# The first half expert's weights beside the last early products, and a new order of token blocks

## The reference, cut to what matters

```python
x = attention(q, k, v, beta)            # reshaped to 3072 tokens x 384
logits = x @ w_gate; P = exp(logits - logits.max())
for _ in range(8):                      # "Sinkhorn rounds"
    P /= P.sum(1, keepdims=True) + 1e-09
    P /= P.sum(0, keepdims=True) + 1e-09
    P *= N / E
for e in range(8):                      # w1[e]: 384 x 1024, w2[e]: 1024 x 384
    out += P[:, e:e+1] * (np.maximum(x @ w1[e], 0) @ w2[e])
h = out @ w_in                          # second layer, 384 x 2048
out = (h * sigmoid(1.702 * h)) @ w_out
```

## Time and profile before

| what | us |
|---|---|
| median of 3 runs (lowest to highest) | 2574.24 (2572.38 to 2574.74) |
| the profiled execution, whole time | 2572.69 |
| its span (first to last instruction) | 2570.9 |
| TensorE busy | 2466.6 (96%) |
| VectorE, ScalarE, GpSimd busy | 1013.1, 663.9, 841.4 |
| share of the last chain on TensorE | 73% |

### The profile page before, as it was taken

One profiled execution on the slowest core, in us unless ns is written; L12 is line 12 of the kernel. 1 busy time (PEld: TensorE's weight loads), 2 busy tenths in 40 slices (PEclk: granted clock), 3 DMA queues, 4 the chain that ended last, 5 costly groups with the idle time before them and its releaser, 6 DMA issues.

```text
span 2570.9 us, 42139 instructions
## 1 busy us (share of the span) xinstructions
PE 2466.6 (96%) x17923; PEld 2362.1 (92%) x17923; DVE 1013.1 (39%) x2181; ACT 663.9 (26%) x1454; POOL 841.4 (33%) x753
## 2 busy tenths in 40 slices
PE   5889999999849999999999999999999999999999
PEld 4778888888749999999999999999999999999999
DVE  5776666663513333333333333333333333333332
ACT  3344444443311111111111111111111122222222
POOL 5545555552060232033113302321331131443432
PEclk9999999999979999999999999999999999999999
DMA  2113323332220111011001101110110010000001
GB/s 78 45 63 102 107 95 108 102 105 75 68 98 2 49 50 32 18 49 50 25 25 50 50 16 35 50 42 8 50 50 25 25 50 1 25 13 13 13 19 56
DMA packets 96378, 124.58 MB, mean 48 GB/s; under 512 B 5184, under 2 KB 82240, under 8 KB 96192
## 3 DMA queue, kind: packets, MB, share of 16 engines
q1 hardware_dynamic: 96192, 121.90, 14.3%
HBM read 91.99 MB, written 29.88 MB: 47 GB/s over the span
## 4 chain that ended last, share of the span: by engine, by line
PE 73%; issue 1%; DMA 1%; POOL 0%; DVE 0%; ACT 0%; SPq 0%; ACTq 0%; DVEq 0%; POOLq 0%
PE bank L1218 39%; PE bank L1189 32%; PE bank L181 1%; PE bank L1121 1%; DMA w_raw<-in_moe_w 0%; PE bank L1167 0%; POOL w_hl L1043 0%; POOL w_hl L1037 0%; DMA h_early<-h_out 0%; DVE h_raw L1327 0%; DVE x_rest L1333 0%; ACT x_rest L1247 0%; PE bank L1107 0%; PE bank L1225 0%; ACT h_out L191 0%
## 5 line engine op out<-in xcount | busy, mean ns | idle before, releaser
L1218 PE MATMUL bank<-w_hl,h_hl 128*128 128x384 f32 x5760 | 1021.5, 334 | 34.1 <-issue 34.1
L1218 PEld LDWEIGHTS bank<-w_hl,h_hl 128*128 128x128 f32 x5760 | 1001.9, 188 | 34.4 <-issue 34.4
L1189 PE MATMUL bank<-x_rest,w_hl 128*128 128x384 f32 x4320 | 783.3, 338 | 0.0
L1189 PEld LDWEIGHTS bank<-x_rest,w_hl 128*128 128x128 f32 x4320 | 763.9, 187 | 0.0
L1371 DVE SCALAR_TENSOR_TENSOR x_tok<-bank,route,x_tok 128x384 f32<-128x384 f32 x384 | 237.2, 618 | 555.5 <-PE bank L1218 555.5
L1072 POOL TENSOR_TENSOR h_hl<-h_raw,h_hl 128x384 fp32r<-128x384 f32 x128 | 125.9, 1016 | 947.8 <-ACT h_hl L1268 947.8
L1276 ACT ACTIVATE h_hl<-bank 128x384 fp32r<-128x384 f32 x384 | 189.0, 492 | 946.0 <-PE bank L1189 946.0
L1349 DVE SCALAR_TENSOR_TENSOR h_hl<-bank,h_hl 128x384 fp32r<-128x384 f32 x384 | 214.2, 558 | 437.6 <-ACT h_hl L1276 437.6
L181 PE MATMUL bank<-x_first,w_hl 128*128 128x384 f32 x1152 | 282.4, 363 | 0.7 <-ACT h_out L191 0.7
L1093 POOL TENSOR_TENSOR h_hl<-h_raw,h_hl 128x384 fp32r<-128x384 f32 x128 | 129.6, 1017 | 296.5 <-ACT h_hl L1286 296.5
L181 PEld LDWEIGHTS bank<-x_first,w_hl 128*128 128x128 f32 x1152 | 188.5, 191 | 11.4 <-issue 10.3
(11 more groups left out here) (116 smaller groups left out, 1813.6 us busy)
## 6 DMA issues: line engine op xcount, KB each, us to landing
w_raw<-in_moe_w SPq DMA_DIRECT2D x48, 768.0 KB, 4.9
h_early<-h_out SPq DMA_DIRECT2D x128, 192.0 KB, 1.9
h_raw<-h_early SPq DMA_DIRECT2D x32, 768.0 KB, 6.1
kq_t<-in_kq_rows SPq DMA_DIRECT2D x48, 256.0 KB, 3.0
kv<-in_kv_cols SPq DMA_DIRECT2D x24, 384.0 KB, 3.9
out<-x_tok SPq DMA_DIRECT2D x8, 576.0 KB, 3.0
w_raw<-in_moe_w_in SPq DMA_DIRECT2D x4, 768.0 KB, 4.6
w_raw<-in_moe_w_out SPq DMA_DIRECT2D x4, 768.0 KB, 4.5
```

The lines of the kernel that those rows point to most:

```text
L1189: m = pe.matmul(bank[:, f, 0:TB], w1_hl[hn % 2][:, a, kc, f * P:(f + 1) * P], x_at(c, kc, b * TB, TB), start=n + kc == 0, stop=n == len(PA ...
L1218: m = pe.matmul(bank[:, 4 + t, 0:DM], h_hl[:, b % 2, a, f, t * P:(t + 1) * P], w2_hl[hn % 2][:, c, f, :], start=n + f == 0, stop=n == len( ...
```

## The change

Three edits belong together.

One: the early `w1` chain gets a seventeenth step. `early_w1_load(16)` fetches half 0's `w1` once more behind store 118, ScalarE and GpSimd split it in thirds beside products 120 to 125, into `w1_hl[0]`. `load_w1(0)`, `high1(0)` and `low1(0)` are gone, and the counts of `pool_w` and `ld_w1` are one lower from there on.

Two: the order of units in a half. Halves 0 to 14 go 2, 3, 0, 4, 1, 5, 6, 7 instead of 0 to 7; half 15 and the quarters keep theirs. All orders and semaphore counts come from one list, `UNITS`, and the place of a unit in it, `AT`, also chooses the hidden buffer (`s % 2` for `b % 2`). TensorE begins with `up(0, 2)`.

Three: in SyncE's queue `load_h(0, 0)` goes ahead of the last early stores, `load_w2(0)` and `load_h(0, 1)` behind them; from half 1 on the order is as it was. On GpSimd the clearing of `x_tok` now stands ahead of `high2(0)` and `low2(0)`. `load_h` waits for the stores of its own block alone.

```diff
-        def early_w1_load(sp, hn):
-            if hn >= E * NH:
+        def early_w1_load(sp, load):
+
+            if load > E * NH:
                 return
-            wait(sp, pool_w1e, KC * hn)
+            hn = load % (E * NH)
+            wait(sp, pool_w1e, KC * load)
...
         def early_w1_high(act, hn, kc):
-            if hn >= E * NH:
+            if hn > E * NH:
...
         def early_w1_low(pool, hn, kc):
-            if hn >= E * NH:
+            if hn > E * NH:
...
+        def block_order(hn):
+
+            if hn >= FFN0 - 1:
+                return list(range(NB))
+            computed = list(range(EB, NB))
+            return computed[:2] + [0] + computed[2:3] + [1] + computed[3:]
+
+        UNITS = [(hn, b) for hn in range(HALVES) for b in block_order(hn)]
+        AT = {unit: s for s, unit in enumerate(UNITS)}
+        COMPUTED = {unit: u for u, unit in enumerate(unit for unit in UNITS if not loaded(*unit))}
+        LOADED = {unit: n for n, unit in enumerate(unit for unit in UNITS if loaded(*unit))}
...
                 def load_w2(hn):
-                    wait(sp, pool_w, 2 * hn + 1)
+                    if hn == 0:
+                        sp.wait_ge(pool_w1e, KC * (FFN0 + 1))
+                    else:
+                        sp.wait_ge(pool_w, 2 * hn)
...
+                load_h(0, 0)
                 for n in range(IN_ATTENTION, EARLY):
                     early_store(sp, n)
                     if n % 8 == 6:
                         early_w1_load(sp, n // 8 + 2)
-
-                for hn in range(HALVES):
+                load_w2(0)
+                for b in range(1, EB):
+                    load_h(0, b)
+
+                for hn in range(1, HALVES):
                     load_w1(hn)
                     load_w2(hn)
...
-                split_half(0)
-
                 pool.wait_ge(pe_xx, len(LATE))
                 pool.memset(x_tok[:, :, :], 0.0).then_inc(pool_zero, 1)
+                high2(0)
+                low2(0)
+
...
                     for f in range(FC):
-                        if u == ups_before(hn) and f == 0:
-                            pe.wait_ge(pool_w, 2 * hn + 1)
+                        if u == 0 and f == 0:
+                            pe.wait_ge(pool_w1e, KC * (FFN0 + 1))
+                        elif u == ups_before(hn) and f == 0:
+                            pe.wait_ge(pool_w, 2 * hn)
...
-                for hn in range(HALVES):
-                    for b in range(NB):
-                        nh, nb = following(hn, b)
-                        back = back_of(hn, b)
-                        if nh < HALVES and not loaded(nh, nb):
-                            up(nh, nb, back)
-                        down(hn, b, back)
+                up(*UNITS[0], None)
+                for s, unit in enumerate(UNITS):
+                    if s + 1 < len(UNITS) and not loaded(*UNITS[s + 1]):
+                        up(*UNITS[s + 1], back_at(s))
+                    down(*unit, back_at(s))
```

More of the change, by code:

```diff
@@ L986, in load_w1 @@
                 def load_w1(hn):
-                    wait(sp, pool_w, 2 * hn)
-                    if hn == 0:
-                        sp.wait_ge(pool_w1e, KC * FFN0)
+                    sp.wait_ge(pool_w, 2 * hn - 1)
                     at = slice(hn % NH * FH, (hn % NH + 1) * FH)
@@ L1005, in load_h @@
                     if hn == 0 and b == 0:
-                        for n in range(4):
-                            sp.wait_ge(st_h[n], 16 * (EARLY // 4))
                         sp.wait_ge(dve_lt, NB)
                         sp.wait_ge(pe_logit, NB)
-                    wait(sp, pool_hlo, FC * (hn * EB + b))
+                    for f in range(FC):
+                        sp.wait_ge(st_h[f], 16 * (EB * hn + b + 1))
+                    wait(sp, pool_hlo, FC * LOADED[hn, b])
                     sp.dma_start(h_raw[:, :, :], h_early[hn, b, :, :, :].rearrange("f p t -> p f t")
                                  ).then_inc(ld_h, 16)
+                load_h(0, 0)
                 for n in range(IN_ATTENTION, EARLY):
@@ L1033, in _, with high @@
             def _(pool):
-                def high(dst, raw, ld, hn):
-                    pool.wait_ge(ld, 16 * (hn + 1))
+                def high(dst, raw, ld, loads):
+                    pool.wait_ge(ld, 16 * loads)
                     _, k, f = raw.shape
@@ L1054, in low1 @@
                 def low1(hn):
-                    low(w1_hl[hn % 2], w1_raw, 2 * hn)
+                    low(w1_hl[hn % 2], w1_raw, 2 * hn - 1)
                 def high2(hn):
                     wait(pool, pe_m2, TT * NB * (hn - 1))
-                    high(w2_hl[hn % 2], w2_raw, ld_w2, hn)
+                    high(w2_hl[hn % 2], w2_raw, ld_w2, hn + 1)
                 def low2(hn):
-                    low(w2_hl[hn % 2], w2_raw, 2 * hn + 1)
+                    low(w2_hl[hn % 2], w2_raw, 2 * hn)
                 def split_half(hn):
@@ L1217, in down @@
                             for n, (a, c) in enumerate(PARTS):
-                                m = pe.matmul(bank[:, 4 + t, 0:DM], h_hl[:, b % 2, a, f, t * P:(t + 1) * P],
+                                m = pe.matmul(bank[:, 4 + t, 0:DM], h_hl[:, s % 2, a, f, t * P:(t + 1) * P],
                                               w2_hl[hn % 2][:, c, f, :], start=n + f == 0,
@@ L1263, in loaded_high @@
                 def loaded_high(hn, b):
-                    wait(act, pe_m2, TT * (hn * NB + b - 1))
-                    act.wait_ge(ld_h, 16 * (hn * EB + b + 1))
+                    s = AT[hn, b]
+                    wait(act, pe_m2, TT * (s - 1))
+                    act.wait_ge(ld_h, 16 * (LOADED[hn, b] + 1))
                     for f in range(FC):
-                        act.copy(h_hl[:, b % 2, 0, f, :], h_raw[:, f, :]).then_inc(act_h, 1)
+                        act.copy(h_hl[:, s % 2, 0, f, :], h_raw[:, f, :]).then_inc(act_h, 1)
                 def relu(hn, b, back):
-                    u = up_index(hn, b)
-                    wait(act, pe_m2, TT * (hn * NB + b - 1))
+                    u, s = COMPUTED[hn, b], AT[hn, b]
+                    wait(act, pe_m2, TT * (s - 1))
                     for f in range(FC):
                         act.wait_ge(pe_m1, FC * u + f + 1)
-                        act.activation(h_hl[:, b % 2, 0, f, :], bank[:, f, 0:TB], ACT.Relu).then_inc(act_h, 1)
+                        act.activation(h_hl[:, s % 2, 0, f, :], bank[:, f, 0:TB], ACT.Relu).then_inc(act_h, 1)
                         if f == 0 and back is not None:
@@ L1299, in sigmoid @@
                             turn_back(back)
[L1301 to L1311, removed]
+                relu(*UNITS[0], None)
+                for s, unit in enumerate(UNITS[1:]):
+                    if loaded(*unit):
+                        loaded_high(*unit)
+                    elif unit[0] < FFN0:
+                        relu(*unit, back_at(s))
+                    else:
+                        sigmoid(*unit, back_at(s))
                 gate_high(FC * NQ * NB - 1)
@@ L1345, in relu_low @@
                 def relu_low(hn, b, back):
-                    s = hn * NB + b
+                    s = AT[hn, b]
                     for f in range(FC):
                         dve.wait_ge(act_h, FC * s + f + 1)
-                        dve.scalar_tensor_tensor(out=h_hl[:, b % 2, 1, f, :], in0=bank[:, f, 0:TB], scalar=0.0,
-                                                 in1=h_hl[:, b % 2, 0, f, :].bitcast(F32), op0=ALU.max,
+                        dve.scalar_tensor_tensor(out=h_hl[:, s % 2, 1, f, :], in0=bank[:, f, 0:TB], scalar=0.0,
+                                                 in1=h_hl[:, s % 2, 0, f, :].bitcast(F32), op0=ALU.max,
                                                  op1=ALU.subtract).then_inc(dve_h, 1)
@@ L1418, in _ @@
                 dve.wait_ge(pool_zero, 1)
[L1419 to L1428, removed]
-                        else:
-                            add_quarter(hn, b)
+                relu_low(*UNITS[0], None)
+                for s, unit in enumerate(UNITS):
+                    if s + 1 < len(UNITS) and not loaded(*UNITS[s + 1]):
+                        if UNITS[s + 1][0] < FFN0:
+                            relu_low(*UNITS[s + 1], back_at(s))
+                        else:
+                            gate(*UNITS[s + 1], back_at(s))
+                    if unit[0] < FFN0:
+                        add_expert(*unit)
+                    else:
+                        add_quarter(*unit)
 def kernel(**inputs):
```

37 lines of the change are left out of this document (17 added, 20 removed).

## The result

The changed kernel takes 2541.02 us (four runs, 2539.44 to 2545.07) against 2574.49 (2572.38 to 2576.87): a ratio of 0.9872, 95% interval 0.9855 to 0.9889, so 33.5 us less. The forecast was 2539.8, in the range 2536 to 2550.

The account below looks back on a forecast made before the run. TensorE was taken as fed except for one 34.1 us pause before `down` and what leads to it; 33.55 + 1.65 - 0.74 = 34.5 us off 2574.24 gives 2539.8 us, range 2536 to 2550.

Parts of the forecast that it names:

- The pause: Before the main part: starting with computed unit `up(0, 2)` lets TensorE begin at 711.99 instead of 745.54, gaining 33.55 us.
- The clock: First 36 matmuls of `down`: without the long wait the granted clock stays full, 7.89 to 6.24, gaining 1.65 us.
- The fetch beside the early products: Early products near 123: ScalarE's wait for half 0's `w1` delays TensorE, costing 0.74 us, between 0 and 1.3.
- the ports: Six new ScalarE and GpSimd pieces beside VectorE's chain: counted as nothing; if exposed, 1.1 us a piece, 3.3 for three.
- rival B: Early stretch: late fetch up to 1.3 and held VectorE pieces up to 3.3, about 4 us less gain, 2543.7; chance 0.12.
- What the memset holds up: Start of main part: memset 709.55 to 717.3, low part done 717.9, 1.2 us to spare; `w2` split by 723.8, 1.6 spare.
- Rival A: Last Sinkhorn round: memset catches L1409, L1414 meets `w2`'s rounding, low part 2.0 us late; time 2541.8; chance 0.13.
- The order of blocks: Halves in the new order: loaded blocks and next half's weights are ready before TensorE wants them; cost zero.
- SyncE's queue: Moved `load_h` and `load_w2` fetches around the last early stores: nothing wanted soon is held up; cost zero.
- C: Interleaved halves: small holes where loaded and computed blocks meet, 0.3 us in each of 15 halves, 4.5 us, 2544.3; chance 0.06.
- D: Next half's weights split too late, each half paying the excess; 3 us excess gives 2584.8, slower than before; chance 0.04.
- E: Some wait keeps `up(0, 2)` behind the clearing and splits, so the pause stays and time is 2574; chance 0.03.

Follow-up runs that it names:

- the old order: Against the changed kernel: early fetch and split of half 0's `w1` kept, but all halves go in order 0 to 7; 2556.85 us.
- the late fetch: Against the changed kernel: new order of units kept, but half 0's `w1` fetched behind the last early store and split after product 127; 2551.03 us.
- the repeated profile: Profile of the changed kernel timed again with nothing changed; median 2541.82 us, main part 1827.4.

## Why the prediction was right, point by point

*The pause.* Predicted 33.55 us; 34.09 before less 0.63 after is 33.46. Shown, and the two halves of the reason by the old order (15.78 us of it come back) and the late fetch (9.71).

*The clock.* Predicted 1.65 us. Shown: without the second hold the main part is 1823.7 against 1825.4: 1.7. In executions with it, the new hole costs 1.85 of waiting and 1.74 of clock (8.10 less 6.36), and that gain is eaten.

*The fetch beside the early products.* Predicted 0.74 us with the ports at nothing. From the third last column sum to the start of relu 127 it was 10.54 us before (700.91 to 711.45), and it is 10.54 again with the late fetch (703.26 to 713.80). In the profile after it is 11.37 (703.85 to 715.22), so 0.83 more. But that one is the exception: in the repeated profile it is 11.94 (702.61 to 714.55), and in every other profile with the fetch and the thirds at this place it is 11.91 to 11.93 too, so 1.4 more. In the repeated profile the 18 matmuls around ScalarE's wait for the fetch take 3.78 us instead of 3.42, and TensorE waits 0.74 for VectorE's row-sum multiply, which takes 1.21 us beside GpSimd's second third. Part of rival B is therefore real. The term that was mis-sized is that of the ports: it was put at nothing and is about 1.0 of the 1.4 us there, because two products to a round did not cover the held instructions; the fetch by itself is the other 0.4. The trace of before had such a hold in the open: in the first round the multiply on L1402 takes 1.47 us from 674.78 beside a GpSimd piece from 674.77, and TensorE waits 2.66 us.

*What the memset holds up.* This step failed. The prediction set L1409 at 709.46 and the memset at 709.55 and concluded that VectorE would be first. In all seven profiles that have the memset at the change's place and the early fetch, VectorE's record does start first, by 0.02 or 0.03 us, and is held all the same. In the profile after, GpSimd's last third ends at 712.57 (711.28 + 1.29), 0.09 behind VectorE's start. A likely reading is that VectorE already stands waiting for that third and GpSimd's next instruction goes ahead of it. The runs show the hold, but not this order of events: with the memset behind the rounds the same instruction also starts before the end of the third (710.81 against 710.89) and takes its usual 0.17 us. Rival A described the hold, down to L1426 meeting the rounding of `w2`. It put the price at 2.0 us; the wait is 1.85, but the clock adds 1.74, so 3.6. And it took the second hold as certain where it is a race: the changed kernel's own three profiles have it twice. So in some executions the last round goes as A said, in others TensorE sees nothing of it, 3.6 us apart in the main part. The sign that the prediction named for A, a low part later than 719, is there in the profile after (723.57, of which 3.75 are the execution's). The three medians of the changed kernel are 2541.02, 2541.82 and 2538.26. That the number held although this step was wrong is luck: A was cheap.

*The sum between marks.* From the first early product of the last stage to the end it is 1902.9 us before (2570.9 - 667.99), and 1871.6, 1872.6 and 1866.4 in the changed kernel's three profiles: 31.3, 30.3 and 36.5 less, where 34.5 were predicted. The first two have the second hold. In the third the first Sinkhorn round also goes 2.7 us better than in the profile before, for reasons outside the change: TensorE waits 1.55 us there and not 2.66, and the next 27 matmuls take 4.98 us and not 6.55. Without that its gain is 33.8, and the steps as measured give 33.46 + 1.7 - 1.4 = 33.8. None of the three is the 33.5 us of the whole times, which mix both outcomes of the race with the scatter.

*The order of blocks, SyncE's queue.* Predicted zero, shown for the order by the run with it in the first half alone (2538.78 us), and for both by no idle row on L1234. Rivals C and D had nothing to stand on; E fell with the 0.63 us.

What isn't shown: which of the runs without a profile lost the race. The scatter of the whole time (before: 2571.6 to 2577.7 on one chip) is as large as the effect. Two sources show in the profiles: the clock in the first 64 us (3.1 of the 3.75 us between the profiles before and after), and the first Sinkhorn round with up to 2.7 us. Whether they are all of it is open.

## What to carry to other kernels

A pause in front of a stage is worth reordering for: find the unit that needs the fewest of the things being prepared, and start with it. When work is pulled forward on GpSimd, look at what VectorE does at that moment and not only at who waits for the result; a long GpSimd instruction of no urgency belongs behind the small operations on the critical chain, or out of the kernel. And where a whole time scatters by more than the step under study, read the step between two marks of the profile: 3.6 us were plain there and lost in the medians.

## What the runs showed of the hardware that was not expected

A held VectorE instruction was not let in between GpSimd instructions that stood ready: 8.13 us behind eight memsets of about 1 us, in the one profile of that kernel. A start 0.02 us ahead in the trace does not mean that an instruction had its ports first (L1421 at 712.48 and the memset at 712.50 against L1426 at 717.56 and the rounding at 717.58, the one held, the other not). And in all three profiles with a wait of 1.8 to 1.9 us in front of `up(0, 3)` the clock fell behind it: in the profile after it is 0.83 over the next ten microseconds and costs 1.74 us on 36 matmuls, about as much as the pause of 34 us had cost. But the length of the wait alone does not decide: in front of the first column sum TensorE waits 2.66 us in nine profiles, and in seven of them the next 27 matmuls take 6.54 to 6.57 us, in the other two (the memset behind the rounds, and the first one without memset) 4.98, which is full speed.
